# Chained attention and two MoE-style layers on one core: x by chunks, and the first expert's first 128 rows fixed a chunk earlier

## The reference, cut to what matters

```python
state = w * state + k_t v_t^T ;  y_t = r_t (state + (u * k_t) v_t^T)      # attention, B=4, H=8, S=768
x = y by token, shape (3072, 384)
xc = x[x @ w_skip > 0]; e = argmax(xc @ w_gate); gate = softmax(...)[e]
out[compute] = xc + gate * (relu(xc @ w1[e]) @ w2[e])                      # F = 1024
h = out @ w_in; g = h * clip(h + 3, 0, 6) / 6; result = g @ w_out          # F = 2048
```

## Time and profile before

| | us |
|---|---|
| median of 3 runs | 698.47 (697.96 to 700.05) |
| the profiled execution | 699.52 |
| its span, first to last instruction | 697.7 |
| PE busy | 686.7 (98%) |
| DVE busy | 381.7 (55%) |
| ACT busy | 323.8 (46%) |
| POOL busy | 141.2 (20%) |

### The profile page before, as it was taken

How to read it: one execution, slowest core, us unless ns; L and a number is a source line. 1 busy time by engine, 2 the same in 40 slices (tenths; PEclk the granted TensorE clock), 3 DMA queues, 4 the chain that set the end, 5 groups by cost and what they waited for, 6 DMA issues and landing times.

```text
span 697.7 us, 13712 instructions
## 1 busy us (share of the span) xinstructions
PE 686.7 (98%) x5072; PEld 623.7 (89%) x5072; DVE 381.7 (55%) x788; ACT 323.8 (46%) x704; POOL 141.2 (20%) x190
## 2 busy tenths in 40 slices
PE   7999999999999999999999999999999999999998
PEld 5888888879999999899999999999999989998997
DVE  5677667678777777666543443343434333434333
ACT  5777777735555555554433333233333333324222
POOL 8757966543232321100000000000000000000000
PEclk9999999999999999999999999999999999999999
DMA  7888876718666668320023004000500050001001
GB/s 137 186 201 198 186 170 153 238 39 294 232 216 211 223 208 279 104 25 1 1 60 32 1 1 84 7 1 0 92 1 0 1 91 1 0 1 47 0 1 45
DMA packets 135161, 65.70 MB, mean 94 GB/s; under 512 B 110724, under 2 KB 130696, under 8 KB 135104
## 3 DMA queue, kind: packets, MB, share of 16 engines
q1 hardware_dynamic: 131088, 60.13, 33.6%
q0 software_dynamic: 2560, 4.60, 2.1%
q10 hardware_dynamic: 1456, 0.20, 0.2%
HBM read 53.37 MB, written 12.48 MB: 94 GB/s over the span
## 4 chain that ended last, share of the span: by engine, by line
PE 94%; DVE 2%; POOL 1%; issue 1%; DMA 1%; ACT 0%; another core or an unknown queue 0%; DVEq 0%; ACTq 0%; POOLq 0%
PE bank_A L1038 8%; PE bank_A L1039 8%; PE bank_A L1037 8%; PE bank_L L1037 4%; PE bank_L L1039 4%; PE bank_L L1038 4%; PE bank_P L1039 4%; PE bank_P L1038 4%; PE bank_P L1037 4%; PE bank_kT L1038 4%; PE bank_kT L1039 4%; PE bank_kT L1037 4%; PE bank_A L954 4%; PE bank_YT L1039 3%; PE bank_YT L1038 3%; PE bank_YT L979 3%
## 5 line engine op out<-in xcount | busy, mean ns | idle before, releaser
L1595 DVE TENSOR_TENSOR g_lo<-g,g_hi 128x512 fp32r<-128x512 f32 x96 | 66.5, 692 | 67.1 <-ACT g_hi L824 67.1
L824 ACT ACTIVATE g_hi<-g 128x512 fp32r<-128x512 f32 x96 | 60.7, 632 | 73.1 <-DVE g L1593 73.1
L1593 DVE SCALAR_TENSOR_TENSOR g<-cut,bank_A 128x512 f32<-128x512 f32 x60 | 41.2, 687 | 76.4 <-ACT cut L821 76.4
L821 ACT ACTIVATE cut<-bank_A 128x512 f32<-128x512 f32 x60 | 35.8, 597 | 94.2 <-PE bank_A L1039 93.7
L1039 PE MATMUL bank_A<-mT_hi,wi_lo 128*128 128x512 f32 x180 | 71.0, 394 | 0.0
L1038 PE MATMUL bank_A<-mT_lo,wi_hi 128*128 128x512 f32 x180 | 70.9, 394 | 0.0
L1037 PE MATMUL bank_A<-mT_hi,wi_hi 128*128 128x512 f32 x180 | 70.0, 389 | 0.0
L658 ACT ACTIVATE bank_A<-ident,own 128x128 f32<-128x128 f32 x188 | 58.1, 355 | 23.7 <-DVE A_sb L1293 18.7
L1593 DVE SCALAR_TENSOR_TENSOR g<-cut,bank_kT 128x512 f32<-128x512 f32 x36 | 24.7, 687 | 67.5 <-ACT cut L821 67.5
L821 ACT ACTIVATE cut<-bank_kT 128x512 f32<-128x512 f32 x36 | 21.5, 597 | 70.5 <-PE bank_kT L1039 70.5
L1037 PE MATMUL bank_kT<-mT_hi,wi_hi 128*128 128x512 f32 x108 | 42.1, 389 | 0.9 <-DVE mT_lo L1586 0.9
(11 more groups left out here) (333 smaller groups left out, 1807.1 us busy)
## 6 DMA issues: line engine op xcount, KB each, us to landing
raw<-in_moe_w_dram SPq DMA_DIRECT2D x24, 512.0 KB
raw<-in_moe_w_dram SPq DMA_DIRECT2D x7, 1536.0 KB
r_in<-in_r_dram SPq DMA_DIRECT2D x24, 192.0 KB, 3.6
v_in<-in_v_dram SPq DMA_DIRECT2D x24, 192.0 KB, 4.2
x_scratch<-y_sb SPq DMA_DIRECT2D x24, 192.0 KB, 2.3
k_in<-in_k_dram SPq DMA_DIRECT2D x23, 192.0 KB, 3.8
m_in<-x_scratch SPq DMA_DIRECT2D x20, 192.0 KB, 5.5
out_dram<-o_sb SPq DMA_DIRECT2D x10, 384.0 KB, 2.8
```

The lines of the kernel that those rows point to most:

```text
L821: eng.activation(cut[f % 2][:, :], p_H[f % 3][:, :], ACT.Relu, bias=0.5, scale=1.0 / 6.0).then_inc(s_cut, 1)
L824: eng.activation(g_hi[f % 4][:, :], g[f % 2][:, :], ACT.Copy).then_inc(s_ghi, 1)
L1593: eng.scalar_tensor_tensor(g[f % 2][:, :], cut[f % 2][:, :], 1.0, p_H[f % 3][:, :], ALU.min, ALU.mult).then_inc(s_g, 1)
L1595: eng.tensor_tensor(g_lo[f % 4][:, :], g[f % 2][:, :], g_hi[f % 4][:, :].bitcast(F32), ALU.subtract).then_inc(s_glo, 1)
```

## The change

x is laid out by chunks (row `(c * 4 + b) * 128`), so that the rows of chunks 0 to 3 are the first 2048; row numbers and the output's addresses follow. The pad is worked out one step earlier, from the count after chunk 3, so the first expert's first 128 ranks hold tokens of chunks 0 to 3 alone. The list is read in two parts: the first 128 ranks once chunk 3 is scattered, ahead of the store of step 21; the rest where the whole list was read. POOL issues the first part's gather ahead of chunk 4's scatters. PE transposes the first part's rows ahead of the last logits, and does the two halves of the first pass on either side of the last count, in place of part of the `go_on` transposes (31 before, 21 after: 2, 2, 5, 4 and 8). ACT's and DVE's orders follow.

```diff
-ON = (8,)
+ON = (2, 5, 4, 8)
...
         def x_rows(b, c):
-            return x_dram[b * S + c * P:b * S + (c + 1) * P, :]
+            return x_dram[(c * B + b) * P:(c * B + b + 1) * P, :]
...
+            def read_list(t):
+
+                for i, done in enumerate(s_slots):
+                    eng.wait_ge(done, 16 * B * len(range(i, NC - TH + t, SETS)))
+                eng.dma_start(listed[:, t, :], slots_by_p[:, t, :]).then_inc(s_listed, 16)
...
+                    if n == NT - 1:
+                        read_list(0)
                     if n > 1:
...
             store(B - 2, NC - 1)
-            for i, done in enumerate(s_slots):
-                eng.wait_ge(done, 16 * B * len(range(i, NC - 1, SETS)))
-            eng.dma_start(listed[:, :, :], slots_by_p[:, 0:TH, :]).then_inc(s_listed, 16)
+            read_list(1)
             store(B - 1, NC - 1)
...
-                eng.dma_start(out[bass.ds(blk * BLK + half * (BLK // 2), BLK // 2), :].rearrange("(t p) n -> p t n", p=P),
-                                  o_sb[:, ts, :]).then_inc(s_out[half], 16)
+                    eng.dma_start(out_rows[ts, bass.ds(blk * P, P), :].rearrange("b p n -> p b n"), o_sb[:, ts, :]).then_inc(s_out[half], 16)
...
-                eng.iota(pairs[c % SETS][:, :, 0:1], [[S, B]], base=c * P, channel_multiplier=1).then_inc(s_id, 1)
+                eng.iota(pairs[c % SETS][:, :, 0:1], [[P, B]], base=c * B * P, channel_multiplier=1).then_inc(s_id, 1)
...
-            scatters(NC - 2, NC - 2, range(B))
...
             for b in range(B):
-                eng.wait_ge(s_st[b], 16 * (NC - b // (B - 1)))
-            rows_of(0, 0, listed, stored=N - P)
+                eng.wait_ge(s_st[b], 16 * (NC - 2))
+            rows_of(0, 0, listed, stored=(NC - 2) * B * P)
+            scatters(NC - 2, NC - 2, range(B))
+            eng.wait_ge(s_listed, 16 * TH)
             scatters(NC - 1, NC - 1, range(0, LATE))
...
-            rows_out(B - 1, NC - 1)
-            exponentials(NC, slice(LATE, B))
...
+            rows_high(0, 0)
+            rows_out(B - 1, NC - 1)
+            exponentials(NC, slice(LATE, B))
             eng.wait_ge(s_raw2, 16 * W2_PARTS)
-            for f in range(G1 - 2):
-                w2_high(f)
-            rows_high(0, 0)
-            for f in range(G1 - 2, G1):
+            for f in range(G1):
                 w2_high(f)
...
-            go_on(5, p_rT)
-            logits_direct(B - 1)
-            x_transposes(B - 1, NC - 1)
-            for b in range(LATE):
-                own_slots(b)
-            go_on(9, p_YT)
-            count(NC, p_countB, LATE, B, 1)
-            go_on(9, p_YT)
-            for b in range(LATE, B):
-                m = own_slots(b)
-            m.then_inc(s_own, 1)
...
+            go_on(2, p_rT)
             half_T(0, 0, 0)
-            go_on(ON[0], p_kT)
+            logits_direct(B - 1)
+            x_transposes(B - 1, NC - 1)
+            for b in range(LATE):
+                own_slots(b)
+            eng.wait_ge(s_gThi, 1)
+            first_half(0, xgT_hi, w1_hi, range(1))
+            go_on(ON[0], p_P)
+            count(NC, p_countB, LATE, B, 1)
             eng.wait_ge(s_rows, NT)
-            eng.wait_ge(s_gThi, 1)
-            first_half(0, xgT_hi, w1_hi)
+            first_half(0, xgT_hi, w1_hi, range(1, 2))
+            go_on(ON[1], p_P)
+            for b in range(LATE, B):
+                m = own_slots(b)
+            m.then_inc(s_own, 1)
+            go_on(ON[2], p_P)
             eng.wait_ge(s_gTlo, 1)
             first_half(0, xgT_lo, w1_hi)
+            go_on(ON[3], p_P)
             first_half(0, xgT_hi, w1_lo, range(1))
             half_T(0, 0, 1)
...
                 if b == 1:
                     eng.wait_ge(s_lt, of + 1)
+                    if c == NC - 1:
+                        eng.tensor_scalar(skip[:, :], p_count[:, B, 0:1], -1.0 / P, 1.0, ALU.mult, ALU.add).then_inc(s_skip, 1)
                     carry(of)
+                    if c == NC - 1:
+                        eng.wait_ge(s_skip, 1)
+                        eng.scalar_tensor_tensor(choice[:, 0, 0:1], skip[:, :], 0.0, choice[:, 0, 0:1], ALU.max, ALU.add).then_inc(s_skip, 1)
+                        eng.wait_ge(s_skip, 2)
...
                 if b == 2 and c == NC - 1:
-                    eng.tensor_scalar(skip[:, :], p_count[:, B, 0:1], -1.0 / P, 1.0, ALU.mult, ALU.add).then_inc(s_skip, 1)
                     carry(c)
-                    eng.wait_ge(s_skip, 1)
-                    eng.scalar_tensor_tensor(choice[:, 0, 0:1], skip[:, :], 0.0, choice[:, 0, 0:1], ALU.max, ALU.add).then_inc(s_skip, 1)
-                    eng.wait_ge(s_skip, 2)
...
-            eng.wait_ge(s_listed, 16)
+            eng.wait_ge(s_listed, 16 * TH)
             eng.tensor_copy(who[0][:, 0, :], listed[:, 0, :])
...
-            route_slot(rts[NC], last, half_B)
-            rt = steps_of(NC + 1)
...
             rows_low(0, 0)
+            route_slot(rts[NC], last, half_B)
+            rt = steps_of(NC + 1)
             split_w1(0, range(1, KC))
```

More of the change, by code:

```diff
@@ L44 @@
 BT = BLK // P
+assert BT == B and NBLK == NC
 LOG_P = P.bit_length() - 1
@@ L447, in load_m @@
                     eng.dma_start(m_in[o * Q:(o + 1) * Q, :, :].rearrange("i k (a j) -> i k a j", j=Q), squares[o]).then_inc(s_m, 16)
+            out_rows = out.rearrange("(b s) n -> b s n", b=B)
             def blocks(blk, i, first=False, last=False):
@@ L457, in blocks @@
                         eng.wait_ge((s_oA, s_oV)[half], blk + 2 + t % (BT // 2))
-                        eng.dma_start(out[blk * BLK + t * P:blk * BLK + (t + 1) * P, :], o_sb[:, t, :]).then_inc(s_out[half], 16)
+                        eng.dma_start(out_rows[t, blk * P:(blk + 1) * P, :], o_sb[:, t, :]).then_inc(s_out[half], 16)
                     return
@@ L544, in _ @@
             eng.iota(token[:, :], [[1, BLK]], base=0, channel_multiplier=0, allow_small_or_imprecise_dtypes=True).then_inc(s_tok, 1)
-            eng.iota(own_rows[:, :, 0:1], [[S, B]], base=(NC - 1) * P - EMPTY, channel_multiplier=1, allow_small_or_imprecise_dtypes=True).then_inc(s_tok, 1)
+            eng.iota(own_rows[:, :, 0:1], [[P, B]], base=(NC - 1) * B * P - EMPTY, channel_multiplier=1, allow_small_or_imprecise_dtypes=True).then_inc(s_tok, 1)
             for t in xg:
```

## The result

The changed kernel takes 704.64 us (median of 6 runs, 698.73 to 706.89); the kernel before, run beside it, 698.88 (6 runs, 697.96 to 700.05).

What follows compares the result with a forecast made beforehand. TensorE (94% of what ended last) was taken as the bound. Skip -0.27, slow half pass +0.56 and PE's lateness -0.68 gave -0.4 us, forecast 698.0 on the 698.47 median; range 697.3 to 699.1, 8-in-10 range 696.3 to 699.8.

Steps and rivals of the forecast that it cites:

- rival D: Expert tiles: padding the first expert from four chunks adds a tile of 17.03 us, 715 us; chance 0.01.
- the skip's wait: PE's wait for y_sb before the x transposes: 0.67 us falls to near 0.4, saving 0.27 us.
- a second half pass: Behind the last count, replacing four go_on: 1.40 us at the low clock, so own slots come 0.56 us later.
- from count to own slots: PE's stretch with the second half pass and five go_on: 2.46 us against 1.90, so +0.56 us.
- The gather's landing: Rows of the first tile's second part land at 153.4; PE's own lateness of 0.68 us against them goes.
- the one before the count: First part's transposes and first half pass replace go_on there; the count waits for DVE anyway, so cost 0.
- Rival B: DVE's remote wait of 2.40 us at 140.54 may shrink: up to 2.4 us more saved, 695.0 to 696.2; chance 0.09.
- Rival C: Lists late on POOL and SP if the first lands after about 135.8: price +2.2 us, 700.6; chance 0.08.
- Cover 1.7 us: Second list lands at 144.7, DVE reads it at 146.36, so its delay behind the early gather costs nothing.
- The sum: Seam up to the second part's transpose at 153.78: -0.27 skip, +0.56 slow half pass, -0.68 PE's lateness: -0.4 us.
- The cover that the prediction quoted: Second tile's low part: DVE ends at 168.63, PE starts at 169.80, so 1.17 us of cover.
- Rival A: Clock stays up until the own slots, ids come 0.3 + 0.27 us earlier: -1.2 us, 697.3; chance 0.22.

Runs made afterwards that it cites:

- the gap: Changed kernel, POOL waiting for PE's last Y between chunk 4's second and third scatters: 1.0055, 1.0093, 1.008; kernel before, waiting ahead of the fourth: 1.007.
- the five comparisons: Five sets of follow-up runs on four chips, each with the kernel before beside its variants; medians of the kernel before 696.91 to 698.44 us.
- the POOL part: Changed kernel with PE's and ACT's orders of the kernel before; layout, skip, early list and early gather kept: 698.01 us (1.0018) and 698.56 us (1.0022).
- the last profile: Changed kernel unaltered, profiled in the fifth set of follow-up runs: span 700.5 us; measured there 702.24 us, 1.0066 of the kernel before.
- the third and fourth comparison: Follow-up sets against the kernel before (697.02 and 696.91 us): changed kernel again, its POOL and SP part, waits among scatters, added go_on; ratios 1.0 to 1.0093.
- the third and the last comparison: Two follow-up sets on the same chip, both timing the changed kernel unaltered against the kernel before: 701.82 us (1.0068) and 702.24 us (1.0066).
- The filled kernel: Changed kernel with nine go_on more behind Y and ten more ahead of the last own slots: 701.11 us, 1.0051 of the kernel before.
- the kernel with the memsets: Kernel before with three waited memsets on POOL ahead of chunk 4's scatters: 699.94 us, 1.0042 of the kernel before.

## Why the prediction was wrong

**Right.** Eight tiles (rival D is out), the skip's wait of 0.40 for 0.67, the times on POOL and SP to 0.3 us but for the early gather (135.68 for 134.9), a second half pass at about 1.4 us (start to start, 149.08 to 150.51), and from count to own slots +0.83 us where +0.56 was priced. The gather's landing took back 0.39, for 0.68 forecast.

**The step that failed first is the one before the count, priced at 0.** It measures +2.75 us: 1.84 up to the last logits (143.49 for 141.65), and 0.91 between them and the count, at the low clock. The prediction reasoned that the count waits for DVE, so what stands ahead of it is free, and that the clock falls, if at all, behind the hole at the count. Instead the hole came behind Y: the copy was 1.84 us later (142.96 for 141.12), and PE had two go_on and three transposes where five go_on stood, and no other work ready. Then logits (1.85 for 1.03), transposes and the first half pass all ran at 1.2 GHz. Sums were ready on DVE at 146.95 (146.71 + 0.24), the count came at 148.37, PE was the late one by 1.4 us. The bound for a half pass at the low level was right; it was applied to the second and not to the first.

**The remote wait was the wrong way round.** Rival B let the 2.40 us wait of the earlier trace rows shrink. The profiles now tie it in time to the row of scatters: the first instruction let go moved by 2.42 us (140.54 to 142.96) as the row's end did (139.52 to 141.94). The prediction moved that row itself, "start near 137.1, the last ends near 142", and asked which lists come late, not what else ended with the row. That the scatters cause the lateness is argued from six profiles with the effect, of which one fits badly, and not shown; the gap was tried only where it does not occur. What held the releases, and on that chip alone, stays open.

**Rival C named the right wait, with the wrong trigger and price.** I gave it 700.6 and 8 in 100, and put its threshold at the first list's landing. The first list was in time, the second read went out as forecast or 1.3 us later (143.1 to 144.5), and DVE had it 1.7 us after that (144.51 to 146.19). "Cover 1.7 us" was counted against DVE's read at 146.36, but that read stood late only because the releases were late. In four of the five comparisons they are not, DVE is ready near 143.7 (145.10 less 1.42 in the last), and there is no cover. What a list later by this costs is bounded by the POOL part, which has the skip and the layout too: 1.0018 and 1.0022, 1.3 and 1.5 us. The Trainium skill (DMA: Bandwidth & Descriptors, Issuing engines are not separate DMA queues) was the reason for C: transfers of all engines share the same 16 DMA engines. For the first list the trace agrees, 2.9 us to landing while they are full. The second landed in 1.7 us, and POOL's issue, 1.28 us for each of four scatters behind the gather, is what made it late.

**The second tile had no term.** The sum ended at 153.78 with "from there PE has no named hole". The second tile's gathers wait for the last scatters, the weights stream beside them, and the cover of its rows before was 1.24 us for the first part and 1.37 for the second (161.17 and 4.2 to landing, PE at 166.74). In the profile after, the second gather went out 4.45 us later (165.62) and took 5.8 us for 4.2, while PE came 3.04 later: less the 1.37 that is 1.6, of which PE shows 1.53. In the last profile it was 3.18, from other terms, as above. The cover that the prediction quoted is that of DVE's low part, one step behind these transposes.

**The sum again**, in the profiled pair: +2.75 before the count, +0.83 to the own slots, -0.39 at the landing, +1.53 at the second tile, +0.1 after: 4.8 of 4.83 us. The forecast's own terms add to -0.39, which makes 698.1 rather than 698.0.

**The clock decides how much a hole costs.** Of the 40 executions of the kernel before in the third and fourth comparison, 26 have a mean clock of 1.0 and take 696.48 to 697.47, 14 have 0.997 or 0.998 and take 697.24 to 699.24. The changed kernel as it is was timed 24 times: once at 1.0 (700.27), else 0.988 to 0.998, and its three best are 698.50, 698.58 and 698.73. Beside the profile after, 0.998 goes with 698.73, 0.993 with 703.07 to 704.98, 0.99 with 706.89. That is more than the slower work alone, by an estimate from these clocks: 0.005 of 702 us is 3.5 us, and the times for 0.993 are 4.3 to 6.3 above. Later ids can also mean the second tile's wait. The Trainium skill (TensorE: Matmul & The Clock Gate, What's actually happening) says the switch moves from run to run; the spread within every kernel agrees. Rival A asked for less, a clock that stays up as far as the own slots. Two of the changed kernel's four profiles meet this, those of the third and the last comparison (own slots at 147.26 and 146.17, clock down from 149.3 and 167.3), and their spans are 698.0 and 700.5, not 1.2 us under the 697.7 of before: the saving did not come with its condition, since the list was late. Over a whole execution the clock stays up nearly never in this kernel, whose largest holes in the seam are 1.36 to 3.7 us, for 1.21 before. The filled kernel keeps it up in 3 of 7 and is then at 697.4 to 697.6, still 0.8 us above the kernel before at full clock on that chip (696.7, the median of 16). The change buys nothing even there: the ids of the second part, not PE's work on the first, set the seam, and it makes their lists later.

## What to carry to other kernels

A cover is measured against a reader; ask first what makes the reader late, since where that goes the cover goes. When a row of DMA issues moves, move with it everything that ends when the row ends, the lists two stages on included. Filler that keeps TensorE busy through a wait can have a price when it is taken out, by the clock, and useful work put in its place helps only if it is not in front of the chain that the wait feeds. A step that comes earlier meets the next cover, so work that out too; look at the spread of the clock over many executions before trusting one profile.

## What was not expected of the hardware

TensorE stayed at 1.2 GHz from 143.0 to 153.3 us while busy without a gap from 143.5 on. Behind holes of 1.21 and 1.40 us the clock fell in one profile each, behind 1.25, 1.36 and 1.52 us it did not; behind or in every hole of 2.3 us and more in the seam and the second tile it did, or was low already, at the latest 2.0 us after the hole's end. Once, in the kernel with the memsets, it fell at 138.3 behind no hole over 0.67 us.

The last releases of TensorE in attention reached the other engines 2.5 to 3.9 us after the end of its instruction on one chip (and in the two first profiles), and promptly on the others, with the same program: ACT's copy at 142.96 and 143.29 behind a Y that ends at 139.4, against 139.42 and 139.52 elsewhere.
